# Attention and two expert layers on one core: transposes in 64-row pairs, prefix counts moved to the next chunk, a second row buffer

## The reference

```python
scores = (1/S) * z @ z.T               # per batch, z is 2496 x 64
x = u * (np.maximum(scores, 0)**2 @ v) # attention without a softmax, times u
# first expert layer: tokens with x @ w_skip > 0 go to the expert of the largest of 8 gate logits
y = gate * (relu(x @ w1[e]) @ w2[e]);  x = x + y   # others keep x
# second expert layer: every token; logits = x @ w_gate2 + bias2[modality]
out = gate * (relu(x @ w1b[e]) @ w2b[e])
```

## Time and profile before

| | |
|---|---|
| three runs, median | 1519.93 us (1517.64 to 1520.74) |
| the profiled execution, its own time | 1518.43 us |
| its span, first to last instruction | 1516.9 us |
| PE busy | 1477.9 us, 97% |
| PEld busy | 1284.2 us, 85% |
| DVE busy | 1010.0 us, 67% |
| ACT busy | 771.3 us, 51% |
| POOL busy | 401.0 us, 26% |
| mean granted clock of PE | 0.994 |
| attention (from start to the last L1422) | about 727 us |

### The profile page before, as it was taken

One profiled execution on the slowest core, in us unless ns is written; L12 is line 12 of the kernel. 1 busy time (PEld: TensorE's weight loads), 2 busy tenths in 40 slices (PEclk: granted clock), 3 DMA queues, 4 the chain that ended last, 5 costly groups with the idle time before them and its releaser, 6 DMA issues.

```text
span 1516.9 us, 34217 instructions
## 1 busy us (share of the span) xinstructions
PE 1477.9 (97%) x11701; PEld 1284.2 (85%) x11701; DVE 1010.0 (67%) x2377; ACT 771.3 (51%) x1504; POOL 401.0 (26%) x379
## 2 busy tenths in 40 slices
PE   8999999999999999999899999999999999999994
PEld 7787888788888888788899999998888888888884
DVE  7989987889779998977766666665333333333331
ACT  6676766667667667666344444444333333333331
POOL 4133312334123433311322222224121221211211
PEclk9999999999999999999999999999999999999997
DMA  5302030201312121200533363322211121111110
GB/s 119 98 30 64 28 99 28 65 30 41 100 32 68 33 58 58 85 30 28 164 109 127 133 213 130 104 95 94 82 47 43 42 71 41 42 53 46 42 48 22
DMA packets 58015, 107.82 MB, mean 71 GB/s; under 512 B 18007, under 2 KB 32354, under 8 KB 57884
## 3 DMA queue, kind: packets, MB, share of 16 engines
q0 software_dynamic: 18464, 58.68, 11.2%
q1 hardware_dynamic: 39420, 47.48, 11.0%
HBM read 75.63 MB, written 32.04 MB: 71 GB/s over the span
## 4 chain that ended last, share of the span: by engine, by line
PE 82%; DVE 5%; issue 5%; DMA 4%; ACT 1%; POOL 1%; SPq 1%; POOLq 0%; ACTq 0%; DVEq 0%
PE pO L1422 24%; PE pS L1668 11%; PE pO L1680 10%; PE pO L1611 9%; PE pS L1628 9%; PE pS L1411 6%; PE pO L1682 5%; PE pM L1668 3%; DVE AH L1077 3%; DMA raw<-in_v_dram 2%; PE pT L1659 1%; DMA token_rows<-xrow,dest 1%; PE pT L1470 1%; DVE AL L1079 1%; DMA A<-token_rows 1%
## 5 line engine op out<-in xcount | busy, mean ns | idle before, releaser
L1079 DVE TENSOR_TENSOR AL<-A,AH 128x512 fp32r<-128x512 f32 (+1 forms) x400 | 318.2, 795 | 13.7
L1422 PE MATMUL pO<-AH,VH 64*128 64x512 f32 (+1 forms) x1520 | 299.9, 384 | 6.7 <-DVE xT L987 4.8
L1422 PE MATMUL pO<-AL,VH 64*128 64x512 f32 (+1 forms) x1520 | 298.7, 383 | 0.0
L1422 PE MATMUL pO<-AH,VL 64*128 64x512 f32 (+1 forms) x1520 | 298.6, 382 | 0.0
L697 ACT ACTIVATE R<-pS 128x512 f32<-128x512 f32 (+1 forms) x400 | 213.2, 588 | 142.0 <-PE pS L1411 141.7
L1077 DVE CAST AH<-A 128x512 fp32r<-128x512 f32 (+1 forms) x400 | 221.1, 553 | 43.7 <-ACT A L706 42.9
L706 ACT ACTIVATE A<-R 128x512 f32<-128x512 f32 (+1 forms) x400 | 228.8, 624 | 15.3 <-DVE AL L1079 15.1
L1680 PE MATMUL pO<-VL,AH 128*128 128x512 f32 x640 | 232.4, 399 | 0.0
L1337 DVE SCALAR_TENSOR_TENSOR AL<-pS,AH 128x512 fp32r<-128x512 f32 x120 | 82.9, 691 | 180.0 <-ACT AH L865 179.9
L1682 PE MATMUL pO<-VL,AL 128*128 128x256 f32 x640 | 179.5, 280 | 0.0
L1422 PEld LDWEIGHTS pO<-AH,VH 64*128 64x128 f32 x1520 | 148.1, 185 | 33.7 <-issue 9.3
(11 more groups left out here) (238 smaller groups left out, 2442.9 us busy)
## 6 DMA issues: line engine op xcount, KB each, us to landing
raw<-in_w_dram POOLq DMA_DIRECT2D x22, 1024.0 KB, 7.8
A<-token_rows SPq DMA_DIRECT2D x21, 536.0 KB, 3.5
uT<-in_u_dram SPq DMA_DIRECT2D x16, 512.0 KB, 3.7
xin<-token_rows SPq DMA_DIRECT2D x24, 268.0 KB, 2.8
raw<-in_v_dram SPq DMA_DIRECT2D x4, 1152.0 KB, 5.9
A<-in_w2t_dram POOLq DMA_DIRECT2D x8, 512.0 KB
raw<-in_v_dram SPq DMA_DIRECT2D x4, 768.0 KB, 7.6
raw<-in_z_dram SPq DMA_DIRECT2D x8, 368.0 KB, 5.0
```

What stands on the lines that cost most here:

```text
L1079: v_.tensor_tensor(AL[k % NBUF][:, 0:n], A[k % NA][:, 0:n], AH[k % NBUF][:, 0:n].bitcast(F32), ALU.subtract).then_inc(al_ready, 1)
L1422: last = t_.matmul(pO[:, (KD * r + d) * QW:(KD * r + d) * QW + n], vv[rows, vo + k * D + d * P:vo + k * D + (d + 1) * P], a[k % NBUF][rows ...
```

## The change

1. `transpose_x` transposes 64 rows at a time instead of 128: for each 128 tokens and each half kd of the features two transposes, one for each half of the array's rows, with a 64 × 64 part of the identity; the lower half goes to bank pT, the upper to columns 0 to 255 of bank pM (`xt_halves`). There are eight a visit instead of four. ACT copies a half chunk with two copies of 256 columns.
2. In `route(g)` the transposes come first, then `prefixes(g - 1)`, moved here from p = 7 of the chunk before, then the gate matmuls. At p = 7 only transposes are left. Chunks 19 and 20 keep their prefixes behind their own transposes. The counts now lie in columns 256 to 335 of pM.
3. As pM is now written by PE and read by ACT and DVE for three purposes, there are new waits: `xrow_half(g, 0)` for lcols_made and base_ready, `pick_experts` and `place_rows` for xrow_copied, `place_rows(g - 1)` for lcols_made of g, `route_rows` for base_ready and the first step of pick_experts.
4. A second row buffer: odd chunks use xkeep, which the first expert layer uses later. rows_stored becomes two semaphores; waits are for the chunk before last.
5. `place_rows(g - 1)` moves on DVE from behind p = 2 to behind p = 5, and on POOL the scatter stands behind the first one or two pieces of v_low, z_low or split_low_first instead of ahead of them all.

```diff
-        prefix = pM[:, 128:128 + (QT + 1) * GR].rearrange("p (t n) -> p t n", n=GR)
+        prefix = pM[:, 2 * P:2 * P + (QT + 1) * GR].rearrange("p (t n) -> p t n", n=GR)
+        xt_halves = [x[:, 0:2 * KD * H].rearrange("p (t k c) -> p t k c", t=2, k=KD) for x in (pT, pM)]
...
+        chunk_rows = [xrow, xkeep[:, :, :, :].rearrange("p b s d -> p (b s) d")]
...
+        def stored_rows(idx):
+            return rows_stored[idx % 2], (STORED if idx % 2 else 0) + 64 * ((idx + 1) // 2)
...
@@ POOL
-                if g > 1:
-                    scatter_chunk(g - 1)
...
+                ahead_of, behind = {QC - 3: ((0, 1), (2, 3, 4)), QC - 2: ((5, 6), (7, 8, 9)), QC - 1: ((0, 1), (2, 3, 4))}.get(c, ((), ()))
+                low = z_low if c == QC - 1 else v_low
                 if b < B - 1:
+                    for n in ahead_of:
+                        low(b + 1, n)
                 if g == (B - 1) * QC + 1:
-                    split_low_first(g)
+                    split_low_first(g, range(0, 1))
+                if g > 1:
+                    scatter_chunk(g - 1)
+                if b < B - 1:
+                    for n in behind:
+                        low(b + 1, n)
+                if g == (B - 1) * QC + 1:
+                    split_low_first(g, range(1, WP))
...
@@ ACT
             def xrow_half(idx, half):
                 act.wait_ge(xt_ready, 2 * idx + half)
-                act.wait_ge(rows_stored, 64 * idx)
-                s_.copy(xrow[:, 2 * half:2 * half + 2, 0:D], pT[:, :].rearrange("p (t d) -> p t d", d=D)).then_inc(xrow_copied, 1)
+                if half == 0:
+                    act.wait_ge(lcols_made, idx)
+                    if idx == CHUNKS:
+                        act.wait_ge(route_step, ROUTE * idx + 1)
+                    act.wait_ge(base_ready, idx)
+                elif idx == CHUNKS - 1:
+                    act.wait_ge(prefix_ready, idx)
+                if idx > 1:
+                    act.wait_ge(*stored_rows(idx - 2))
+                to = chunk_rows[idx % 2][:, 2 * half:2 * half + 2, 0:D].rearrange("p t (k r c) -> p r t k c", k=KD, r=2)
+                for r in range(2):
+                    ins = s_.copy(to[:, r, :, :, :], xt_halves[r])
+                ins.then_inc(xrow_copied, 1)
...
@@ DVE
             def row_meta(idx):
-                dve.wait_ge(rows_stored, 64 * idx)
+                if idx > 1:
+                    dve.wait_ge(*stored_rows(idx - 2))
...
             pick_experts:
                 dve.wait_ge(lcols_made, idx)
+                if idx < CHUNKS:
+                    dve.wait_ge(xrow_copied, 2 * idx + 1)
...
             place_rows:
                 dve.wait_ge(prefix_ready, idx)
+                if idx < CHUNKS - 1:
+                    dve.wait_ge(lcols_made, idx + 1)
+                dve.wait_ge(xrow_copied, 2 * idx + 2)
...
+                if idx > 1:
+                    dve.wait_ge(*stored_rows(idx - 1))
...
-                        if p == 2 and g > 1:
+                        if p == 5 and g > 1:
                             place_rows(g - 1)
...
@@ PE
                 for i in range(2):
                     for kd in range(KD):
-                        last = t_.transpose(pT[:, (2 * i + kd) * P:(2 * i + kd + 1) * P], xT[:, kd, (2 * half + i) * P:(2 * half + i + 1) * P], ident[:, :])
-                return last
+                        for r, rows in enumerate(halves):
+                            last = t_.transpose(xt_halves[r][:, i, kd, :], xT[rows, kd, (2 * half + i) * P:(2 * half + i + 1) * P], ident[rows, rows])
+                last.then_inc(xt_ready, 1)
...
             route:
-                pe.wait_ge(base_ready, idx)
+                pe.wait_ge(base_ready, idx - 1 if 1 < idx < CHUNKS else idx)
+                transpose_x(idx, 0)
+                if 1 < idx < CHUNKS:
+                    prefixes(idx - 1)
                 (the 16 gate matmuls)
-                transpose_x(idx, 0).then_inc(xt_ready, 1)
...
             route_rows:
-                transpose_x(idx, 1).then_inc(xt_ready, 1)
+                pe.wait_ge(base_ready, idx)
+                pe.wait_ge(route_step, ROUTE * idx + 1)
+                transpose_x(idx, 1)
...
                             route_rows(g)
-                            prefixes(g)
+                            if g == CHUNKS - 1:
+                                prefixes(g)
...
+            pe.wait_ge(xrow_copied, 2 * CHUNKS + 2)
             prefixes(CHUNKS)
-            pe.wait_ge(xrow_copied, 2 * CHUNKS + 2)
```

More of the change, by code:

```diff
@@ L58 @@
 STORED = 64
+ROUTE = 15
 def bass_attention_two_moe(nc, u, v, z, w_skip, w_gate, w1, w2, modality, w_gate2, bias2, w2t, out):
@@ L224, in bass_attention_two_moe @@
         meta_ready = sem("meta_ready")
-        rows_stored = sem("rows_stored")
+        rows_stored = [sem(f"rows_stored{i}") for i in range(2)]
         final_step = sem("final_step")
@@ L494, in split_low, with split_low_first @@
                     ins.then_inc(wl_ready, 1)
-            def split_low_first(g):
-                for n, (raw, wh, wl) in enumerate(weight_pieces(0)):
+            def split_low_first(g, pieces):
+                for n in pieces:
+                    raw, wh, wl = weight_pieces(0)[n]
                     wait(wh_ready, n + 1)
@@ L514, in _ @@
             pool.wait_ge(consts_made, 3)
-            for n, semaphore in enumerate((rows_stored, PH[0].stored, PH[1].stored)):
+            for n, semaphore in enumerate((rows_stored[1], PH[0].stored, PH[1].stored)):
                 pool.dma_start(xs[GR * CAP + n * P:GR * CAP + (n + 1) * P, :], pad_row[:, :]).then_inc(semaphore, STORED)
@@ L993, in row_meta @@
             def row_meta(idx):
-                dve.wait_ge(rows_stored, 64 * idx)
-                v_.tensor_copy(xrow[:, :, TOK:TOK + 3], meta[:, ds(4 * idx, 4), :]).then_inc(meta_ready, 1)
+                if idx > 1:
+                    dve.wait_ge(*stored_rows(idx - 2))
+                v_.tensor_copy(chunk_rows[idx % 2][:, :, TOK:TOK + 3], meta[:, ds(4 * idx, 4), :]).then_inc(meta_ready, 1)
             def pick_experts(idx):
@@ L1032, in step @@
                     dve.wait_ge(route_step, n[0])
-                v_.tensor_copy(xrow[:, :, LOGITS:LOGITS + E], lg[:, :, 1, :])
+                v_.tensor_copy(chunk_rows[idx % 2][:, :, LOGITS:LOGITS + E], lg[:, :, 1, :])
                 dve.wait_ge(exp_done, idx)
@@ L1039, in set_gates @@
                 step(v_.tensor_tensor(gates[:, :, :], gates[:, :, :], take[:, :, :], ALU.mult))
-                v_.tensor_tensor(xrow[:, :, GATE], gates[:, :, 0], gates[:, :, 1], ALU.add).then_inc(route_step, 1)
+                v_.tensor_tensor(chunk_rows[idx % 2][:, :, GATE], gates[:, :, 0], gates[:, :, 1], ALU.add).then_inc(route_step, 1)
             def place_rows(idx):
@@ L1483, in route @@
                 last.then_inc(lcols_made, 1)
-                transpose_x(idx, 0).then_inc(xt_ready, 1)
             def route_rows(idx):
-                transpose_x(idx, 1).then_inc(xt_ready, 1)
+                pe.wait_ge(base_ready, idx)
+                pe.wait_ge(route_step, ROUTE * idx + 1)
+                transpose_x(idx, 1)
             def prefixes(idx):
                 pe.wait_ge(onehot_ready, idx)
-                t_.matmul(pM[:, 128:128 + (QT + 1) * GR], before[:, :], oh[:, :, :].rearrange("p t g -> p (t g)"), start=True, stop=False)
+                t_.matmul(pM[:, 2 * P:2 * P + (QT + 1) * GR], before[:, :], oh[:, :, :].rearrange("p t g -> p (t g)"), start=True, stop=False)
                 for i in range(QT):
```

21 lines of the change are left out of this document (6 added, 15 removed).

## The result

| | before | after |
|---|---|---|
| median of six runs each | 1520.26 us (1517.64 to 1520.74) | 1525.01 us (1522.55 to 1525.96) |
| ratio after to before | | 1.0029, 95% interval [1.002, 1.0039] |
| the profiled execution: span, its own time | 1516.9, 1518.43 us | 1524.4, 1525.96 us |
| mean granted clock of PE | 0.994 | 0.992 |

The changed kernel is slower by 0.29%, and the interval leaves out 1. The forecast was 1513, range 1504 to 1519: wrong, on the other side.

The account below looks back on a forecast made before the run. PE was taken to bound the attention, with DVE nearly full in some chunks. Terms 8.85 + 1.7 - 2.4 - 0.9 - 0.85 = 6.4 us took the profiled 1518.43 to 1512.0, median 1513; range 1504 to 1519 (8 in 10).

Parts of the forecast that it names:

- PE's prices: PE's side trips: 0.055 us a transpose pair, 0.275 for p = 7, 1.25 for p = 3; gain 0.75 a chunk.
- Rival 1: PE's transposes: weight loads take turns, 0.11 us a pair; gain 0.38 a chunk, 1516.5 us on the profiled execution; chance 0.17.
- rival 4: PE's transposes: a pair has no overlap, 0.22 us; PE loses 0.52 a chunk, 1528 us in all; chance 0.05.
- The chunks that PE sets: Attention chunks where PE's gain counts in full: ten at 0.75 us, 7.5; with g = 1 and 19, 8.85.
- (a): DVE's place_rows behind p = 5 waits for its chunk's gate matmuls: 0.8 us in three c = 4 chunks, 2.4.
- (c): POOL in c = 2: scatter issues between second and third VL piece make the fifth late, 0.3 × 3 = 0.9 us.
- Waits added: New waits and delays on DVE, ACT, POOL, PE and at the attention's end: 2.4, 0.9 and 0.85 us lost, elsewhere nothing.
- (b): ACT's first xrow half waits for base, relus of p = 7 behind it: 0.7 us later, covered by three steps of lead.
- The third rival: DVE becomes the bound through place_rows' wait: 1.5 us net in ten chunks of c = 4, 0, 1; 1529 us; chance 0.08.
- Waits removed: ACT's 24.0 us of waiting for the scatter to land goes; two waits reached PE (g = 5, 10): gain 1.7 us.
- (e): End of attention: place_rows(19) waits for both ACT copies, delaying scatter 19 and the first MoE load: cost 0.85 us.

Follow-up runs that it names:

- place6_copy7: Changed kernel with place_rows behind p = 6 instead of p = 5 on DVE and ACT's first row copy behind p = 7 instead of 6: 1514.02 us, ratio 0.9994.
- place6: Changed kernel with place_rows on DVE behind p = 6 instead of p = 5: 1524.42 us, ratio 1.003.
- old_pe_place5: Kernel before with second row buffer, place_rows behind p = 5 and POOL's new order, PE's order as before: 1520.14 us, ratio 1.0005.
- pieces_first: Changed kernel with all five POOL pieces of c = 2, 3 and 4 ahead of the scatter: 1512.28 us, ratio 0.9987.
- pairs_pool_order: Kernel before with second row buffer, 64-row pairs and POOL's new order; prefixes at p = 7, place_rows at p = 2: 1507.4 us, ratio 0.9954.
- old_pe_place5_wait: old_pe_place5 with place_rows also waiting for its own chunk's lcols_made, PE's waits moved to suit: 1524.71 us, ratio 1.0031.
- two_buffers: Kernel before with the second row buffer alone: 1516.44 us, ratio 0.9972.
- the warm version: pairs_pool_order with 80 filler matmuls on PE behind the last prefixes: 1504.74 us, ratio 0.9933.
- scatter_first: Changed kernel with the scatter ahead of all POOL's pieces again: 1549.12 us, ratio 1.0224.

## Why the prediction was wrong, point by point

**PE's prices were right.** In g = 11 of the changed kernel, against the earlier trace rows:

```profile
423.13 0.41 PE L1450 MATMUL pO<-AL,VH 64*128 64x512 f32 x2
423.37 0.21 PE L1499 MATMUL pT<-ident,xT 64*128 64x64 f32 x1
423.39 0.21 PE L1499 MATMUL pM<-ident,xT 64*128 64x64 f32 x1
423.42 0.22 PE L1499 MATMUL pT<-ident,xT 64*128 64x64 f32 x1
...
424.52 0.50 PE L1439 MATMUL pS<-ZH 64*128 64x512 f32 x2
424.86 0.40 PE L1439 MATMUL pS<-ZL,ZH 64*128 64x512 f32 x2
```

A pair starts every 0.06 us (0.055 taken); the trip costs 424.52 - 423.36 + 0.11 = 1.27 (1.25 worked out). At p = 7 of the same chunk:

```profile
438.05 0.39 PE L1450 MATMUL pO<-AL,VH 64*128 64x512 f32 x2
...
438.50 0.48 PE L1439 MATMUL pS<-ZH 64*128 64x512 f32 x2
438.81 0.40 PE L1439 MATMUL pS<-ZL,ZH 64*128 64x512 f32 x2
```

The next pair could start at 438.28; the scores start 0.22 later, and their second pair 0.08 late: 0.31 for 0.275. Rival 1 (loads in turn) and rival 4 (no overlap) fall with these rows: two loads are recorded in every 0.06 us, though one is recorded as 0.14 us long, so they overlap. The Trainium skill's page "TensorE: Matmul & The Clock Gate", section "LDWEIGHTS (loading the stationary operand)", prices one load by its columns, whatever its rows. The earlier trace rows agree for one load, but the sum by the count of loads, 0.86 us a chunk, did not come.

**The chunks that PE sets were right.** c = 0 and 1 with g = 17 and 18 were to gain 0.75 each and two ACT waits, 6.95 us; they gained 7.0. DVE's wait at rank, up to 3.43 us against the 2.2 worked out, costs nothing there, as said:

```profile
424.72 0.23 DVE L1078 TENSOR_TENSOR rank<-pM,base 128x64 f32<-128x64 f32 x1 [3.43 <-PE pM L1513]
```

**The step that failed is the pair of terms (a) and (c) under "Waits added", and with (a) the "covered" of (b).** I priced place_rows' wait by itself, 0.8 us in c = 4 only, and POOL's order by how late its fifth piece would be, 0.3 in c = 2. By those terms c = 2, 3, 4 and g = 16 together were to come out at +0.9 - 2.25 + 2.4 + 0 = +1.05 us. They came out at +11.9. Of the 13.9 us between the sum (1512.0) and the profiled execution (1525.96), that is 10.9. Three things were wrong in it:

- c = 3 stood among the chunks that gain in full. But DVE is nearly full there, too (31.82 us busy of 34.10 in g = 3 of the kernel before), and the new order costs.
- Term (a) looked for who is queued behind place_rows on DVE, not for what place_rows lets go: base, for which ACT's row copy waits ahead of the relus of p = 7, and dest, for which the scatter waits. (b) said "covered by three steps of lead"; place6_copy7 against place6, 0.9994 against 1.003, says that it wasn't.
- Term (c) counted where the pieces stand in POOL's program, not when they run. A late scatter holds back all that is behind it; ACT goes on making high parts, and the pieces then run in a row, with DVE standing for the whole of it. The earlier trace rows had that mechanism and its price, 4.68 us for a split. I used it only for c = 4, and took the new order to thin it out. It was the place that mattered, more than the count: in the kernel before three in a row ran in each chunk of c = 2, 3 and 4, and PE was idle for only 0.5 us in the c = 4 window; two in a row cost DVE 3.1 us at p = 7, right behind up to 3.5 at rank. old_pe_place5 shows the late scatter without the wait: about 0.3%.

What each is worth, by ratios to the kernel before: pieces first 0.42% (1.0029 to 0.9987), the place of place_rows and of the copy 0.24% more (0.9987 to 0.9963). Taken in the other order it is 0.35% for the places (1.0029 to 0.9994) and 0.31% for the pieces, so the shares hold to about a tenth of a per cent. What is left, 0.9963 against the 0.9954 of pairs_pool_order, is within the intervals. So as far as the intervals tell, the two causes account for the loss, and moving the prefixes itself was worth nothing measurable beside what its later base and dest cost. Whether 45 us of waiting at rank would cost anything by itself, with the run of pieces gone and the copy moved, was not tried separately: place6 changes both the wait and the time of base. The 4.6 us of old_pe_place5_wait are not its price either, since the place of the long operations changed with it (lsh 12.6 to 29.5 us).

**The third rival had the right side and the wrong place.** It put the loss into c = 4, 0 and 1, up to 1.5 us in each of ten chunks. c = 0 and 1 lost nothing; c = 3 and 4 lost 1.0 to 1.2 us each and g = 16 lost 2.2. In c = 2 it is 1.1 on the mean, but the three windows, with finer bounds, changed by 0.8, -0.5 and 2.6, and why they differ is open. It is not the second half of v: ACT takes it up 20.5 to 21.6 us after the gate matmuls before and 20.5 to 20.9 after. The losses lie where DVE's idle time in a chunk is smaller than the wait and the run together; that this decides, and not the lead at p = 5, is argued.

**Waits removed** look undersized: 1.7 us taken, 0.28% or 4 us measured by two_buffers; the part in c = 0 was right (1.9).

**The end, (e), 0.85 us, was 3.8**, the other 2.95 of the 13.9. (g = 1 and 19 gave 1.2 us where 1.35 was worked out.) The chain that ended last, before and after:

```profile
733.66 3.30 DMA xin<-token_rows
...
737.01 0.66 PE pT L1558 x4
```

```profile
738.58 4.70 DMA xin<-token_rows
743.33 1.12 PE pT L1592 x4
...
744.87 1.72 PE pO L1574 x32
```

What (e) priced was about right: from PE's last transposes of g = 19 to scatter 19 it is 3.58 us for 2.92, 0.66 more. The rest I had not counted. From there to the first MoE transposes it is 2.0 us more, 1.4 of them the load of x, 4.70 us for 3.30. From these to the second set it is 1.15 more (9.27 for 8.12), at a mean granted clock of 0.84 for 1.00; PE had stood idle for 4.0 us at the load, and for 1.7 before. What the clock costs at this place is shown by the warm version. That the change brings it is not: two_buffers, without any of (e)'s waits, has 0.84 there as well, and 25.6 us for the 22.5 of before. Why the load is longer is open. In the nine kernels with 64-row pairs it takes 4.4 to 5.4 us and the scatter of chunk 20 is issued while it runs; in the five without them it takes 2.9 to 3.6, and that scatter starts at most 0.4 us before its end.

## What to carry to other kernels

For an operation that is moved later, follow what it releases as far as the next engine's queue, and not only what stands behind it: here base and dest, whose followers had time to spare in one chunk and none in the next. Work that waits in a queue behind a late instruction does not vanish but bunches; if it excludes another engine while it runs, as POOL's pieces do DVE, put it ahead of the wait, where its own producer spaces it out. And take a change apart: the second buffer, the pairs and POOL's order come to 0.9954, and with a filler that keeps PE busy to 0.9933 [0.992, 0.9947], while with the moved prefixes it was 1.0029. Last, when an operation grows, look whether another shrank: the 29.4 us of lsh looked like a new cost, and DVE's busy time had not changed.

## What the runs showed of the hardware

- Two 64 × 64 transposes in different halves of the array's rows start 0.02 us apart in g = 11 of the changed kernel, pair after pair every 0.06 us, with a load of 0.14 us for each; whole ones with 128 moving columns started every 0.11.
- A DVE operation on 64 columns (0.22 us) took 3.29, 5.76 and 6.95 us when two, four and five subtractions of 128 × 512 ran on POOL: in each case to within 0.1 us of the end of POOL's run. It had begun 0.6 us or so before the first subtraction (147.88 and 148.53 in scatter_first), while the scatter's last DMA was being issued; 11 such operations that met only the scatter's issues, in the changed kernel, took 0.22 to 0.23. Starts on POOL are rough in the profile, so when the standing begins is not known.
- Over g = 2 to 18 DVE was busy for 530.75 us before, 529.50 after and 520.72 in pieces_first, while its ten longest operations moved from the splits into pick_experts, and all but one of them out again.
- After 5.8 us without work PE had the lower clock (1.2 GHz) for part of the next 9.2 us, mean granted 0.81, in pairs_pool_order, and four transposes took 1.12 us for 0.66.
